# Keys and values by thirds of kv's rows in 8 KB runs, with tile 0 scored on two thirds ahead of the last; queries in 2 KB runs

## The reference

```python
kv_pool = kv.reshape(B, H // 4, 4, W // 4, 4, C).mean(axis=(2, 4))   # kv: 1 x 384 x 32 x 128
k = v = kv_pool.reshape(B, -1, C) @ w_sr                             # 768 x 128
s = (q @ k.transpose(0, 2, 1)) / np.sqrt(C)                          # q: 1 x 12288 x 128
a = np.exp(s - s.max(-1, keepdims=True)); a /= a.sum(-1, keepdims=True) + 1e-09
x = a @ v
h = x @ w_in;  x = (h * (1 / (1 + np.exp(-1.702 * h)))) @ w_out      # 128 -> 2048 -> 128
h = x @ w_in2; return (h * np.clip(h + 3, 0, 6) / 6) @ w_out2
```

## Time and profile before

| | |
|---|---|
| median of 3 runs | 1280.79 us |
| the profiled execution | 1280.32 us, its span 1278.6 us |
| TensorE busy | 1270.0 us (99%), granted clock 1.00 |
| VectorE busy | 1034.1 us (81%) |
| ScalarE busy | 1027.4 us (80%) |
| GpSimd busy | 34.4 us (3%) |
| DMA | 65.69 MB, 51 GB/s over the span |

### The profile page before, as it was taken

The page is one execution under the profiler, slowest core; times in us unless marked ns, Lnnn a source line. Parts: engine busy times, 40 slices in busy tenths (PEclk is TensorE's granted clock), DMA queues, the critical chain, the costliest instruction groups (busy, mean ns, idle before and its releaser), DMA issues.

```text
span 1278.6 us, 18310 instructions
## 1 busy us (share of the span) xinstructions
PE 1270.0 (99%) x5800; PEld 1055.4 (83%) x5800; DVE 1034.1 (81%) x1084; ACT 1027.4 (80%) x1216; POOL 34.4 (3%) x46
## 2 busy tenths in 40 slices
PE   8999999999999999999999999999999999999998
PEld 7888888888888888888888888888888888888887
DVE  5788887888878878888788888887888878887768
ACT  3888877888788888887788878888888778887776
POOL 1800000000000000000000000000000000000000
PEclk9999999999999999999999999999999999999999
DMA  8421321303213123032130220311303213022001
GB/s 280 126 44 40 75 46 28 74 9 65 57 17 74 30 44 74 0 74 49 25 74 13 60 63 11 74 34 40 74 0 74 49 25 74 18 47 67 1 9 17
DMA packets 183685, 65.69 MB, mean 51 GB/s; under 512 B 104560, under 2 KB 176368, under 8 KB 183408
## 3 DMA queue, kind: packets, MB, share of 16 engines
q1 hardware_dynamic: 182576, 65.30, 22.3%
q10 hardware_dynamic: 1088, 0.13, 0.1%
HBM read 22.87 MB, written 6.34 MB: 23 GB/s over the span
## 4 chain that ended last, share of the span: by engine, by line
PE 97%; SPq 1%; DMA 1%; DVE 0%; ACT 0%; issue 0%; DVEq 0%
PE pair L1082 14%; PE pair L1083 14%; PE pair L1086 14%; PE bank_av L1082 9%; PE bank_av L1083 9%; PE bank_av L1086 9%; PE bank_out L1086 7%; PE bank_out L1083 7%; PE bank_out L1082 7%; PE score_banks L1086 2%; PE score_banks L1083 2%; PE score_banks L1082 2%; DMA kv_sb<-in_kv_dram 1%; SPq L354 0%; SPq L362 0%; SPq L366 0%
## 5 line engine op out<-in xcount | busy, mean ns | idle before, releaser
L912 DVE TENSOR_TENSOR mid_lo<-work,mid_hi 128x1024 fp32r<-128x1024 f32 (+1 forms) x193 | 233.9, 1212 | 112.5 <-ACT mid_hi L628 112.4
L1082 PE MATMUL pair<-x_hi,w_hi 128*128 128x512 f32 (+1 forms) x774 | 300.7, 388 | 0.0
L1083 PE MATMUL pair<-x_hi,w_lo 128*128 128x512 f32 (+1 forms) x774 | 300.0, 388 | 0.0
L1086 PE MATMUL pair<-x_lo,w_hi 128*128 128x512 f32 (+1 forms) x774 | 299.9, 387 | 0.0
L589 ACT ACTIVATE work<-pair 128x1024 f32<-128x1024 f32 x184 | 189.2, 1028 | 120.8 <-PE pair L1086 118.5
L904 DVE SCALAR_TENSOR_TENSOR work<-work,pair 128x1024 f32<-128x1024 f32 (+1 forms) x194 | 232.9, 1201 | 15.3 <-ACT work L616 14.6
L891 DVE TENSOR_TENSOR mid_lo<-work,mid_hi 128x1024 fp32r<-128x1024 f32 x184 | 223.6, 1215 | 25.1 <-ACT mid_hi L604 25.0
L616 ACT ACTIVATE work<-pair,half 128x1024 f32<-128x1024 f32 (+1 forms) x194 | 213.1, 1099 | 4.3 <-PE pair L1086 4.2
L628 ACT ACTIVATE mid_hi<-work 128x1024 fp32r<-128x1024 f32 (+1 forms) x193 | 201.8, 1046 | 2.3 <-DVE work L904 2.3
L604 ACT ACTIVATE mid_hi<-work 128x1024 fp32r<-128x1024 f32 x184 | 194.7, 1058 | 1.6
L1082 PEld LDWEIGHTS pair<-x_hi,w_hi 128*128 128x128 f32 x774 | 145.3, 188 | 33.7 <-ACT work L589 4.2
(11 more groups left out here) (175 smaller groups left out, 1560.2 us busy)
## 6 DMA issues: line engine op xcount, KB each, us to landing
p_keys<-p_turned SPq DMA_DIRECT2D x368, 96.0 KB, 2.2
inv_b<-inv_dram SPq DMA_DIRECT2D x23, 256.0 KB, 3.2
out_dram<-y_sb SPq DMA_DIRECT2D x92, 64.0 KB, 2.4
q_raw<-in_q_dram SPq DMA_DIRECT2D x88, 64.0 KB, 2.0
kv_sb<-in_kv_dram SPq DMA_DIRECT2D x6, 768.0 KB, 9.4
w_raw<-in_moe_w_in_dram SPq DMA_DIRECT2D x2, 1024.0 KB, 8.0
kv_sb<-in_kv_dram SPq DMA_DIRECT2D x6, 256.0 KB, 8.1
inv_dram<-inv_t SPq DMA_DIRECT2D x92, 0.5 KB
```

What stands on the lines that cost most here:

```text
L912: dve.tensor_tensor(in_pair(mid_lo[mid2(t, p)], t, p, c), in_pair(act2[p % 2], t, p, c), in_pair(mid_hi[mid2(t, p)], t, p, c), ALU.subtrac ...
L1082: pe.matmul(dst, a_hi, b_hi, start=start, stop=False)
L1083: pe.matmul(dst, a_lo, b_hi, start=False, stop=False)
L1086: return pe.matmul(dst, a_hi, b_lo, start=False, stop=stop)
```

## The change

kv is cut by its rows instead of its columns: chunk a holds rows 128a to 128a+127, one row on each partition, and so 256 keys. It comes in two transfers of 1 MB per chunk, four groups of columns each, and the last half of the third in 512, 256 and 256 KB; a run is 8 KB (4 and 2 KB in these last). Of each 1 MB piece VectorE adds three groups and GpSimd the fourth. The parts of keys are 256, 256, 128 and 128. Tile 0's scores are made by thirds (`scores_first`), in score banks laid out so that the first two thirds of a slot are contiguous; their maximum is taken early, and joined with that of the last third. Slot 0's high part moves from ScalarE to VectorE. The order of each engine's list changes. Tile 0's and tile 1's queries come in 2 KB runs, four tokens on a partition, so that their copies from PSUM step in fours; tile 1's are issued without a wait. The diagonal matrices stand ahead of weight piece 1. `keys_of(n)` now also waits for the low part of the keys of part n-1, `values_of(1)` for q_lo, `values_of(2)` for v_lo(0). The diff, cut to its core (deleted functions and PSUM layouts are left out):

```diff
-    q_first = q[:, 0:TILE].rearrange("b (s p) c -> p (b s) c", p=128)
-    q_second = q[:, TILE:2 * TILE].rearrange("b (a s i) c -> i (b a) s c", a=4, i=32)
+    q_first = q[:, 0:TILE].rearrange("b (p j) c -> p (b j c)", j=4)
+    q_second = q[:, TILE:2 * TILE].rearrange("b (a s i j) c -> s a i (b j c)", a=4, s=4, j=4)
...
-    kv_cols = kv.rearrange("b (p a) (g w) c -> p (b g) a (w c)", a=KV_ROWS, w=R)
+    kv_chunks = kv.rearrange("b (a p) w c -> a p (b w c)", p=128)
...
+        def first_scores_at(s, n):
+            if n == CHUNKS - 1:
+                return s * KEYS + (2 * CHUNK_KEYS if s % 2 == 0 else 0)
+            return s * KEYS + n * CHUNK_KEYS + (0 if s % 2 == 0 else CHUNK_KEYS)
...
-            sp.wait_ge(kv_row_loaded[ROW_GROUPS - 1][0], 16)
+            def load_kv(a, first, groups, loaded):
+                src = kv_chunks[a][:, first * R * C:(first + groups) * R * C]
+                at = (a * KV_GROUPS + first) * R * C
+                sp.dma_start(kv_sb[:, at:at + groups * R * C], src).then_inc(loaded, 16)
+            load_kv(0, 0, 4, kv_loaded[0])
+            sp.dma_start(w_sr_sb[:, :], w_sr).then_inc(w_sr_loaded, 16)
+            load_kv(0, 4, 4, kv_loaded[1])
+            sp.dma_start(q_raw[:, :], q_first).then_inc(q0_loaded, 16)
+            load_kv(1, 0, 4, kv_loaded[2])
+            load_kv(1, 4, 4, kv_loaded[3])
+            load_kv(2, 0, 4, kv_loaded[4])
+            load_kv(2, 4, 2, kv_last_loaded[0])
+            load_kv(2, 6, 1, kv_last_loaded[1])
+            load_kv(2, 7, 1, kv_last_loaded[2])
+            for n in range(4):
+                sp.dma_start(q_raw1[32 * n:32 * (n + 1), :], q_second[n]).then_inc(q1_loaded, 16)
...
+            def add_fourth(n):
+                at = (n * 4 + 3) * R * C
+                group = kv_sb[:, at:at + R * C]
+                hold(kv_loaded[n], 16)
+                pool.tensor_tensor(group[:, 0:2 * C], group[:, 0:2 * C], group[:, 2 * C:4 * C],
+                                   ALU.add).then_inc(fourth_half_added, 1)
+                hold(fourth_half_added, n + 1)
+                pool.tensor_tensor(group[:, 0:C], group[:, 0:C], group[:, C:2 * C],
+                                   ALU.add).then_inc(fourth_added, 1)
+            for n in range(5):
+                add_fourth(n)
...
-                if piece == 2:
+                if piece == 1:
...
+            q_high_first()
             pooled_copy(0)
             k_hi_copy(0)
-            q_high_first()
             v_hi_copy(0)
             pooled_copy(1)
+            k_hi_copy(1)
+            v_hi_copy(1)
             pooled_copy(2)
-            k_hi_copy(1)
             k_hi_copy(2)
-            v_hi_copy(1)
+            v_hi_copy(2)
+            pooled_copy(3)
+            k_hi_copy(3)
+            v_hi_copy(3)
             q1_copy()
             exponential(0, 0)
             exponential(0, 1)
-            p_hi_first(0)
             exponential(0, 2)
             p_hi_first(1)
             exponential(0, 3)
...
+            def add_last_pixels(n):
+                first, count = ((4, 2), (6, 1), (7, 1))[n]
+                at = ((CHUNKS - 1) * KV_GROUPS + first) * R * C
+                groups = kv_sb[:, at:at + count * R * C].rearrange("p (g n) -> p g n", g=count)
+                dve.wait_ge(kv_last_loaded[n], 16)
+                dve.tensor_tensor(groups[:, :, 0:2 * C], groups[:, :, 0:2 * C], groups[:, :, 2 * C:4 * C],
+                                  ALU.add).then_inc(kv_last_added, 1)
...
+            def early_maximum(m):
+                if m == 0:
+                    dve.wait_ge(early_scored, 1)
+                else:
+                    dve.wait_ge(scores_ready, SLOTS)
+                for s in (2 * m, 2 * m + 1):
+                    at = first_scores_at(s, 0)
+                    dve.reduce_max(early_max[:, s:s + 1], score_banks[:, at:at + WIDE], AX_X,
+                                   negate=True).then_inc(max_part_ready, 1)
+            def late_maximum(m):
+                dve.wait_ge(scores_ready, 2 * m + 2)
+                at = first_scores_at(2 * m, CHUNKS - 1)
+                late = score_banks[:, at:at + 2 * CHUNK_KEYS].rearrange("p (s n) -> p s n", s=2)
+                dve.reduce_max(late_max[:, 2 * m:2 * m + 2], late, AX_X, negate=True).then_inc(max_part_ready, 1)
+                dve.wait_ge(max_part_ready, 3 * m + 3)
+                dve.tensor_tensor(neg_max[:, 2 * m:2 * m + 2], early_max[:, 2 * m:2 * m + 2],
+                                  late_max[:, 2 * m:2 * m + 2], ALU.min).then_inc(max_ready, 2)
+            def p_hi_first():
+                dve.wait_ge(pt_ready, 1)
+                dve.tensor_scalar(first_in_chunks(p_high, 0), turned_in(0), 1.0, None,
+                                  ALU.mult).then_inc(pt_hi_first_ready, 1)
...
-            for g in range(KV_GROUPS - ROW_GROUPS):
-                add_pixels(g)
+            add_pixels(0)
+            add_pixels(1)
+            q_low_first()
+            add_pixels(2)
             k_lo_part(0)
-            add_row_pixels(KV_GROUPS - 2, 0)
-            add_row_pixels(KV_GROUPS - 2, 1)
-            q_low_first()
-            add_row_pixels(KV_GROUPS - 2, 2)
-            add_row_pixels(KV_GROUPS - 1, 0)
-            add_row_pixels(KV_GROUPS - 1, 1)
-            add_row_pixels(KV_GROUPS - 1, 2)
             v_lo_part(0)
+            add_pixels(3)
             k_lo_part(1)
+            add_pixels(4)
+            v_lo_part(1)
+            add_last_pixels(0)
             k_lo_part(2)
-            maximum(0, 0)
-            v_lo_part(1)
-            maximum(0, 1)
-            maximum(0, 2)
+            add_last_pixels(1)
+            add_last_pixels(2)
+            v_lo_part(2)
+            early_maximum(0)
+            k_lo_part(3)
+            v_lo_part(3)
+            late_maximum(0)
+            early_maximum(1)
+            late_maximum(1)
+            p_hi_first()
             p_lo_first(0)
-            maximum(0, 3)
             p_lo_first(1)
+            inverse_first()
             maximum(1, 0)
-            inverse_first()
             p_lo_first(2)
...
+            def pool_half(n):
+                a, first = n // 2, n % 2 * 4
+                if n >= 2 and first == 0:
+                    pe.wait_ge(pooled_ready, a)
+                pe.wait_ge(kv_added, n + 1)
+                for g in range(3):
+                    pool_pixels(a, first + g, 1)
+                pe.wait_ge(fourth_added, n + 1)
+                last = pool_pixels(a, first + 3, 1)
+                if first == 4 or a == CHUNKS - 1:
                     last.then_inc(kv_pooled, 1)
+            def pool_last(n):
+                if n == 0:
+                    pe.wait_ge(pooled_ready, 3)
+                pe.wait_ge(kv_last_added, n + 1)
+                for g in ((4, 5), (6,), (7,))[n]:
+                    last = pool_pixels(CHUNKS - 1, g, 2)
+                if n == 2:
+                    last.then_inc(kv_pooled, 1)
...
+            keep_busy(7)
+            pool_half(0)
+            keep_busy(3)
+            pool_half(1)
+            keep_busy(1)
+            turn_q_first(0)
             pe.wait_ge(w_sr_loaded, 16)
             keys_of(0)
+            keep_busy(1)
+            pool_half(2)
             values_of(0)
             pe.wait_ge(k_lo_ready, 1)
             pe.wait_ge(q_lo_ready, 1)
+            for s in range(SLOTS):
+                scores_first(s, 0)
+            pool_half(3)
             keys_of(1)
+            values_of(1)
+            pe.wait_ge(k_lo_ready, 2)
+            scores_first(0, 1)
+            scores_first(1, 1).then_inc(early_scored, 1)
+            scores_first(2, 1)
+            scores_first(3, 1)
+            pool_half(4)
+            pool_last(0)
             keys_of(2)
+            values_of(2)
+            pool_last(1)
+            pool_last(2)
+            keys_of(3)
+            values_of(3)
             pe.wait_ge(k_hi_ready, PARTS)
+            pe.wait_ge(v_lo_ready, 3)
+            scores_first(0, 2, low=(k_lo_ready, PARTS))
+            scores_first(1, 2).then_inc(scores_ready, 2)
             turn_q_first(1)
+            scores_first(2, 2)
+            scores_first(3, 2).then_inc(scores_ready, 2)
+            pe.wait_ge(v_lo_ready, PARTS)
             pe.wait_ge(q1_copied, 1)
             turn_probs(0)
             turn_probs(1)
+            pe.wait_ge(q_lo_ready, 2)
+            pe.wait_ge(exp_ready, 3)
+            scores_second(0)
             pe.wait_ge(pt_lo_ready, 1)
             turn_probs(2)
             turn_probs(3)
             weigh_first(0)
             pe.wait_ge(pt_lo_ready, SLOTS - 1)
+            scores_second(1)
             spread_first_inv()
+            pe.wait_ge(pt_lo_ready, SLOTS + 1)
+            scores_second(2)
             pe.wait_ge(exp_ready, SLOTS + 1)
+            scores_second(3)
```

More of the change, by code:

```diff
@@ L227, in attention_and_two_ffns @@
         w_sr_loaded = sem("w_sr_loaded")
[L228 to L229 removed]
+        kv_loaded = [sem(f"kv_loaded{n}") for n in range(5)]
```

(30 more changed lines are left out.)

213 lines of the change are left out of this document (81 added, 132 removed).

## The result

The changed kernel took 1291.85 us (median of 1291.63, 1292.06, 1287.09 and 1292.33) beside 1280.59 us for the kernel before: a ratio of 1.0079, 95% interval [1.0067, 1.0092] (the ratio weighs every run, the one at 1287.09 too, so it lies below that of the medians). It is slower, as forecast, and by more: 11.3 us, where the forecast was 7. The profiled execution took 1291.63 us, its span is 1289.9 us, which is 11.3 us longer than the span before. One run of e8_fill_q further down, at 3562.87 us, is in a slow state and is left out of its median.

The account below looks back on a forecast made before the run. TensorE's unbroken stream was taken as the bound, so only its start counted: 7.4 us later, less 0.3 for closing gaps, +7.1 us on 1280.32 or 1280.79, stated as 1287.5 us; range 1282.5 to 1292.

Parts of the forecast that it names:

- The order of VectorE's list: VectorE's subtractions wait for TensorE and ScalarE between pieces' additions; the last k_hi at 33.05 us, 8.3 us later.
- the three signs of being wrong: VectorE's idle time mainly kv's DMA; second piece landing outside 9.3 to 12 us; granted clock below 1.00 between 20 and 40.
- the clock's rival: TensorE's clock falls to half during the start: +4 to +6.5 us, 1292 to 1294; chance 0.13.
- the shorter end: From the last k_hi to the stream's start, early scores and maxima save 0.95 us: 5.65 us instead of 6.6.
- the landing of piece 1: Two new kv pieces and w_sr in by 10.9 us, bounds 9.3 and 11.9, before VectorE's additions start.
- against it: no gap is long, and the fillers stay: Argument that TensorE's clock would hold at the start, with gaps of up to 1.2 us.
- k_lo waits: VectorE waits for ScalarE's k_hi ahead of its k_lo subtractions: 2.7 and 2 us.
- GpSimd's fourth group: GpSimd's additions for each kv piece, 1.2 to 1.4 us, hide beside VectorE's 1.55 us.
- Strided reads of PSUM: Copies of tile 0's queries stepping through PSUM taken at 0 extra; 1.3 us kept for the range.
- GpSimd's weights: GpSimd's fifth weight split ready at about 52.2 us, wanted at 53.5; if late, some 1 us at most.
- The same case: At the start, half the stalls hidden under landings, the saved 2.9 us pay the rest: 1278 to 1283; chance 0.07.
- the faster case: Kv's landings set the start's pace, VectorE passing its waits without delay: 2.9 us saved, 1277.4; chance 0.08.

Follow-up runs that it names:

- e8_fill_q: e1 with VectorE's subtraction for tile 0's q_lo moved behind the additions of piece 2: 1285.09 us, ratio 1.0038 to the kernel before.
- e1: The changed kernel with some 22 more filler matmuls in TensorE's waits, the other engines' lists untouched: 1286.30 us, ratio 1.0047 to the kernel before.
- e2: The changed kernel with VectorE's list alone reordered, each piece's additions ahead of the subtraction that waits for ScalarE: 1282.83 us, ratio 1.0025 to the kernel before.
- e11: e9 with each 1 MB piece of kv in two 512 KB transfers in runs of 2 KB: 1281.47 us, ratio 1.0012 to the kernel before.
- e12: e9 run once more, in the same rounds and on the same chip as e11: 1280.07 us, ratio 1.0000 to the kernel before.
- e10: The changed kernel run once more, unaltered, in five rounds: 1290.41 us, ratio 1.0080 to the kernel before.
- e5: The changed kernel with VectorE's and TensorE's lists rewritten, early maxima taken sooner and a few fillers: 1281.10 us, ratio 1.0005 to the kernel before.
- e6: e5 with the fourth group of each 1 MB piece added by VectorE instead of GpSimd: 1281.11 us, ratio 1.0006 to the kernel before.
- e9: e5 without the fillers that stood in TensorE's way and with fewer at two other places: 1279.86 us, ratio 0.9992 to the kernel before.
- e3: The changed kernel with VectorE's list reordered, fillers added, and piece 4's pooling moved ahead on TensorE: 1283.32 us, ratio 1.0023 to the kernel before.

## Why the prediction was right, and where not

**Right: the bound, the place and the sign.** Only the start of the stream moved, and span less start stayed the same. The order of VectorE's list costs as the forecast said: e1 keeps its cost at full clock, and e2 takes most of it out (4.1 of 5.9 us). The rest went with TensorE's list and the fillers, which the forecast had not priced apart.

**The number is in part luck.** Two of the three signs of being wrong that I had named came in: piece 1 was there by 9.17 us, outside 9.3 to 12, and the clock fell between 20 and 40 us. The third did not: most of VectorE's idle time is put down to ScalarE. The forecast's own terms reach from 1285.5 to 1290, and 1291.85 lies outside; it lies in the range that I gave, up to 1292, because half of the clock's rival had been taken into it. And two misses run against each other: piece 1 landed earlier, which took off about 1.5 us, and the clock added 5.5.

**The order's size, step by step, read from e1,** since the forecast assumed a full clock. Start of q_lo: forecast 15.3, e1 13.71. k_lo(1): 24.5, 23.08. k_lo(2): 29.9, 28.25. Last k_hi: 32.7, 30.90. Stream: 38.7, 36.84. The difference is 1.4 to 1.9 us throughout, and 1.6 of it is there at the first step. From q_lo to the last k_hi the forecast has 17.4 us and e1 17.2; from the last k_hi's end (33.05, 31.18) to the stream 5.65 and 5.66. So the round trips and the shorter end were sized well, and the mis-sized term is the landing of piece 1: forecast 10.9 (bounds 9.3 to 11.9), measured 9.17 in the changed kernel, 8.95 in e1. From 0 to 9.6 us the queue moved 306 GB/s after, against 231 in the earlier trace rows, and from 9.6 to 17.7 us 396 against 369. I had let 8 KB runs bring 10% at most, and that only later. e11 shows their part in the early pace: with 2 KB runs it had 272 GB/s in the first window, e12 with 8 KB runs 305. What raised it from 231 to 272 wasn't tried. Of the 1.95 us that piece 1 came earlier in e1, 0.4 went to slower additions (below).

With e1's stream start the sum would have been 1280.8 + 5.5 - 0.3 = 1286.0. I said 1287.5; the one run of the changed kernel with a clock of 0.998 took 1287.09.

**Wrong: that the clock would stay.** The step is the clock rival's "against it: no gap is long, and the fillers stay". It got 0.13, and it came in three of the four first runs and, at 0.993 to 0.997, in all five of e10. Its price, +4 to +6.5 us, was right (5.5 by e1), though it had been scaled from the first six passes of the earlier trace rows, where the granted clock reads 1.00; that half the clock doubles a pass is shown only by the eight pooling passes above, 0.97 and 1.91 us. Its time, 1292 to 1294, meets 1291.85 nearly, but on top of an order's part that was 1.5 us too large. The fillers do stay, but they were laid for another pace: behind piece 1 the changed list has single fillers for waits of 1.1 us. I weighed the longest gap only, and not how much less TensorE would do in the stretch: 2.35 of 3.40 us against 7.23 of 8.10 before. The likeliest case was order plus clock, as eight of the nine runs of the changed kernel show (0.992 to 0.997; the ninth, 0.998).

**k_lo waits.** I wrote 2.7 and 2 us for VectorE's waits for k_hi. After shows 4.11 and 3.85, e1 2.76 and 2.36: the surplus is the half clock. Under it TensorE does the pooling and the keys ahead of the first, and ahead of the second the twelve score passes as well: they end at 28.26 us, and the pooling of piece 4 stands behind them, though its additions were done at 26.74.

**GpSimd's fourth group** was costed at nothing, beside VectorE at 1.2 to 1.4 us. It isn't free. GpSimd's timeline of after, the first step beside VectorE's additions, then with VectorE waiting:

```profile
6.63 1.39 POOL L498 TENSOR_TENSOR kv_sb<-kv_sb 128x256 f32<-128x256 f32 x1 [3.78 <-DMA kv_sb<-in_kv_dram]
...
17.44 0.72 POOL L498 TENSOR_TENSOR kv_sb<-kv_sb 128x256 f32<-128x256 f32 x1 [0.44 <-DMA kv_sb<-in_kv_dram]
```

And VectorE's second step, beside GpSimd and alone:

```profile
7.48 0.97 DVE L817 TENSOR_TENSOR kv_sb<-kv_sb 128x384 f32<-128x384 f32 x1
...
20.19 0.56 DVE L817 TENSOR_TENSOR kv_sb<-kv_sb 128x384 f32<-128x384 f32 x1
```

That is 0.4 us more for VectorE's additions of piece 1, 1.97 us where I had 1.55, on the chain to q_lo. Piece 2 pays it again, beside GpSimd's addition for piece 3, which starts at 14.95 us; pieces 3 and 4 take 0.56:

```profile
15.73 0.96 DVE L817 TENSOR_TENSOR kv_sb<-kv_sb 128x384 f32<-128x384 f32 x1
```

e5 and e6 together say that the share is worth nothing even so: what VectorE is spared in elements it pays in waiting.

**Strided reads of PSUM** cost nothing, as taken: q_hi 0.60, q_lo 0.69, q_t 0.60 us, beside 0.60 and 0.68 in the earlier trace rows. **GpSimd's weights** were in time: from 43 to 100 us none of TensorE's waits is for GpSimd. **The same case and the faster case** are out: the first needs two round trips under a landing, and none was; the second is nearest to what e9 built, with hardly a wait for ScalarE left, and that took 1279.9, not 1277.4.

## What to carry to other kernels

In an in-order engine's list, put work whose input has landed ahead of anything that waits for a round trip through two other engines (here 4.1 us of 1286). In the trace the fault shows as an instruction whose data have long landed and that has no wait of its own, right behind one that waits. When a change lengthens waits around a TensorE that is only just kept warm, compare its busy time by windows before and after, not only its longest gap, and expect to lay the fillers anew. And price a filler's own place: those of e3 and e5 held the clock and cost about 1 us each (the wait of 0.94; and e5's stream at 31.86 us against e9's at 30.44).

## What the runs showed of the hardware

- The granted clock fell from 2.4 to 1.2 GHz in a stretch where TensorE had been busy 2.35 of 3.40 and 2.29 of 3.44 us with no idle time over 1.2 us. The same kernel fell for 6.8 us in one profiled run and 17.1 in another; e9's list kept it in 11 of 11 runs, and in 10 of 12 as e12. In e9 TensorE was busy 2.83 of 3.40 us in the window 11.8 to 15.2.
- Additions of fp32 in SBUF on VectorE and GpSimd at once do not overlap in full: 0.56 becomes 0.97 us, 0.72 becomes 1.39. The Trainium skill (SBUF — State Buffer, SBUF: two separate sides) says that a VectorE operation with two SBUF inputs and a GpSimd operation that reads SBUF take turns at a shared port, each for its whole length. The rows agree roughly: GpSimd's step starts at 6.63 us and ends at 8.02, which is 0.57 behind the end of VectorE's first (7.45), and VectorE's second ends 0.43 behind that.
- Between 9.6 and 15 us kv came at 429 GB/s in 8 KB runs and 1 MB transfers, and at 393 in 2 KB runs and 512 KB transfers, in otherwise the same kernel.
- 256 KB of queries in 512-byte runs, issued behind kv's last rows, held the last of these up by 1.1 us in the profiled run.
